# Splitting the first token load by halves of the heads, and the front of an attention and two-MoE kernel

## The reference, cut to what matters

```
scores = scale * x @ state.T            # (8, 8, 512, 32)
a  = softmax over states;  xread = a @ state
a2 = softmax over tokens of scores.T;  sread = a2 @ x
x  = concat(xread, sread)               # 4608 rows of 512
g  = h * clip(h + 3, 0, 6) / 6,  h = x @ w_in;   y = g @ w_out
out = per row: gate * eom * (relu(y @ w1[e]) @ w2[e]),  e = argmax of y @ w_gate
```

## Time and profile before

| | |
|---|---|
| median of 3 runs | 1136.63 us (1136.08 to 1137.5) |
| the profiled execution, its own time | 1139.21 us |
| its span, first to last instruction | 1137.5 us |
| PE busy | 1108.3 us, 97% |
| DVE, ACT, POOL busy | 58%, 42%, 7% |
| mean granted TensorE clock | 0.991 |

### The profile page before, as it was taken

The page is one execution under the profiler, slowest core; times in us unless marked ns, Lnnn a source line. Parts: engine busy times, 40 slices in busy tenths (PEclk is TensorE's granted clock), DMA queues, the critical chain, the costliest instruction groups (busy, mean ns, idle before and its releaser), DMA issues.

```text
span 1137.5 us, 20219 instructions
## 1 busy us (share of the span) xinstructions
PE 1108.3 (97%) x6199; PEld 875.9 (77%) x6200; DVE 659.0 (58%) x1269; ACT 477.0 (42%) x789; POOL 74.7 (7%) x95
## 2 busy tenths in 40 slices
PE   9999999999999999999999997889999999999996
PEld 7777777777777777777777986777888888878885
DVE  6574655565645646546565454775566645657642
ACT  4454434444443444444444444334344423435420
POOL 0000100100001001001000010100111101010011
PEclk9999999999999999999999998999999999999998
DMA  9210211111102101111004088649977754785641
GB/s 366 100 38 1 75 38 37 38 38 54 59 1 75 38 3 73 38 38 38 1 10 121 2 289 261 202 130 279 277 232 228 223 171 140 224 273 175 177 146 60
DMA packets 129794, 135.59 MB, mean 119 GB/s; under 512 B 13999, under 2 KB 107823, under 8 KB 127152
## 3 DMA queue, kind: packets, MB, share of 16 engines
q1 hardware_dynamic: 95056, 87.26, 24.8%
q10 hardware_dynamic: 28896, 29.36, 8.4%
q0 software_dynamic: 5760, 17.90, 4.2%
HBM read 90.06 MB, written 45.47 MB: 119 GB/s over the span
## 4 chain that ended last, share of the span: by engine, by line
PE 86%; DVE 4%; DMA 3%; issue 2%; ACT 2%; SPq 1%; ACTq 1%; DVEq 0%; POOL 0%; POOLq 0%
PE y_ps L962 32%; PE h_ps L944 16%; PE y_ps L1036 15%; PE h_ps L1012 8%; PE y_ps L1012 7%; PE a_ps L919 3%; PE h_ps L934 2%; DMA raw_first<-in_w 2%; ACT we L1209 1%; DMA xg<-buckets 1%; PE a_ps L817 1%; PE a_ps L903 1%; PE a_ps L883 1%; DMA out<-yo,out_row 1%; PE b_ps L825 1%
## 5 line engine op out<-in xcount | busy, mean ns | idle before, releaser
L962 PE MATMUL y_ps<-w_out_hi,hid_hi 128*128 128x512 f32 x512 | 204.7, 400 | 0.0
L962 PE MATMUL y_ps<-w_out_hi,hid_lo 128*128 128x512 f32 x512 | 199.7, 390 | 0.0
L962 PE MATMUL y_ps<-w_out_lo,hid_hi 128*128 128x512 f32 x512 | 199.4, 389 | 0.0
L1036 PE MATMUL y_ps<-we,act_t_hi 128*128 (+1 forms) x608 | 188.6, 392 | 5.1 <-DVE act_t_lo L1632 2.9
L944 PE MATMUL h_ps<-att_hi,mix 128*128 128x512 f32 x512 | 184.1, 403 | 0.1
L1547 DVE SCALAR_TENSOR_TENSOR hid<-hid,h_ps 128x512 f32<-128x512 f32 x128 | 87.7, 685 | 144.8 <-ACT hid L1157 144.8
L1157 ACT ACTIVATE hid<-h_ps,three 128x512 f32<-128x512 f32 x128 | 87.9, 687 | 150.4 <-PE h_ps L944 150.3
L1036 PEld LDWEIGHTS y_ps<-we,act_t_hi 128*128 128x128 f32 x608 | 114.8, 189 | 29.8 <-issue 5.9
L962 PEld LDWEIGHTS y_ps<-w_out_hi,hid_hi 128*128 128x128 f32 x512 | 96.1, 188 | 49.2 <-issue 30.4
L1555 DVE TENSOR_TENSOR hid_lo<-hid,hid_hi 128x512 fp32r<-128x512 f32 x128 | 88.1, 688 | 62.8 <-ACT hid_hi L1164 62.3
L1036 PE MATMUL y_ps<-we,act_t_lo 128*128 (+1 forms) x304 | 119.0, 392 | 0.0
(11 more groups left out here) (249 smaller groups left out, 1517.8 us busy)
## 6 DMA issues: line engine op xcount, KB each, us to landing
raw<-in_w ACTq DMA_DIRECT2D x12, 2048.0 KB, 10.4
hid_mv<-hidden SPq DMA_DIRECT2D x148, 128.0 KB
hidden<-expert_hid SPq DMA_DIRECT2D x70, 256.0 KB
xg<-buckets SPq DMA_DIRECT2D x156, 64.0 KB
xb<-in_x_rows SPq DMA_DIRECT2D x8, 1024.0 KB, 5.0
x_t<-in_x_t SPq DMA_DIRECT2D x7, 1024.0 KB, 4.9
buckets<-pad_row SPq DMA_DIRECT2D x8, 774.0 KB
w_in_raw<-in_w_in SPq DMA_DIRECT2D x4, 1024.0 KB, 13.3
```

The costliest lines, as they stand in the source:

```text
L962: i = pe.matmul(y_ps[:, t, :], hid_of(b, j)[1 + hp][:, t * P:(t + 1) * P], w_out_s[wp][:, j, :], start=(j == 0 and m == 0), stop=(j == KF ...
L1036: i = pe.matmul(y2_ps[:, slot % 2, :], act_t[hp][:, slot % 2, f, :], we[:, bass.ds(w_at + (wp * WPART + KD * F + f * DM), DM)], start=(f = ...
```

## The change

The 1 MB load of the first batch's tokens becomes two loads of 512 KB, one for partitions 0 to 63 (heads 0 to 3) and one for partitions 64 to 127 (heads 4 to 7), with the load of the states between them. The first batch's scores are issued group by group: the four matmuls of group 0 after the first half's load, raising a new semaphore `s1_first`, then the four of group 1 after the second half's load, raising `s1_ps`. TURN 0 of the first batch waits for `s1_first` in place of `s1_ps`. WARM_START goes from 60 to 44 matmuls. Other batches' scores keep their order.

```diff
-    WARM_START, WARM = 60, {0: 75, 3: 55, 8: 30}
+    WARM_START, WARM = 44, {0: 75, 3: 55, 8: 30}
...
-        load_x_t(0)
+        sp.dma_start(x_t[0:D], x_t_dram[0, 0:D]).then_inc(sem("x_t_first"), 16)
         sp.dma_start(keys_of(0), keys[0]).then_inc(sem("first_keys_loaded"), 16)
+        sp.dma_start(x_t[D:2 * D], x_t_dram[0, D:2 * D]).then_inc(sem("x_t_loaded0"), 16)
         load_in(0)
...
+                    x_of = keys_t(a)
+                    if a == 0:
+                        pe.wait_ge(sem("first_keys_loaded"), 16)
+                        for g in range(GROUPS):
+                            pe.wait_ge(sem(("x_t_first", "x_t_loaded0")[g]), 16)
+                            for q in range(H // GROUPS):
+                                i = pe.matmul(bank_ap(g)[NS * q:NS * q + NS, :], keys_of(a)[D * g:D * g + D, q, :],
+                                              x_of[D * g:D * g + D, q, :], start=True, stop=True)
+                            i.then_inc(sem(("s1_first", "s1_ps")[g]), 1)
+                        continue
                     wait(pe, f"x_t_loaded{a % 2}", 16 * (a // 2 + 1))
-                    if a == 0:
-                        pe.wait_ge(sem("first_keys_loaded"), 16)
-                    else:
-                        pe.wait_ge(sem(f"keys_loaded{a // half_b}"), 16)
-                    x_of = keys_t(a)
+                    pe.wait_ge(sem(f"keys_loaded{a // half_b}"), 16)
...
                 elif name == "TURN":
-                    wait(dve, "s1_ps", a + 1)
+                    if a == 0 and n == 0:
+                        dve.wait_ge(sem("s1_first"), 1)
+                    else:
+                        wait(dve, "s1_ps", a + 1)
```

More of the change, by code:

```diff
@@ L873, in side @@
                             wait(pe, *free)
-                    wait(pe, f"x_t_loaded{a % 2}", 16 * (a // 2 + 1))
+                    x_of = keys_t(a)
                     if a == 0:
                         pe.wait_ge(sem("first_keys_loaded"), 16)
-                    else:
-                        pe.wait_ge(sem(f"keys_loaded{a // half_b}"), 16)
-                    x_of = keys_t(a)
+                        for g in range(GROUPS):
[5 more added lines that the diff above has]
+                        continue
+                    wait(pe, f"x_t_loaded{a % 2}", 16 * (a // 2 + 1))
+                    pe.wait_ge(sem(f"keys_loaded{a // half_b}"), 16)
                     for q in range(H // GROUPS):
```

## The result

Six runs of the changed kernel have a median of 1142.13 us (1139.76 to 1145.29), six of the kernel before 1136.58 (1136.08 to 1137.7). The ratio is 1.0047, 95% interval 1.0035 to 1.0060: 0.47% slower, which is 5.3 us of 1136.58; the two medians are 5.55 apart. The forecast was 1137.9 with a range up to 1139.5, so the result is slower than the range allows.

The account below looks back on a forecast made before the run. PE, busy for 97% of the span, was taken to bound the kernel; group 1's scores 1.44 later less 0.16 of slack gave +1.28 on the median 1136.63, so 1137.9 us, whole range 1135.6 to 1139.5.

Parts of the forecast that it names:

- The stretch that matters: The first 24 us of the chain that ended last, claimed to be the only stretch the change touches.
- a front shift is carried to the end: PE has no idle time from 25 to 640 us, so a shift of its start there is carried on whole.
- a load to half the partitions moves about 220 GB/s: First token halves, 64 partitions each: 524 kB take 2.38 us at 220 GB/s, against 1.36 at the full 385.
- PE's path: Front of PE's program: group 1 and the warm-ups queued behind it start 1.44 later, first layer at 20.04 instead of 18.60.
- the landing of the first half: First token load at the front: first half and states land at 5.37, which is 4.60 plus 0.77 for the slower rate.
- the sum: Whole kernel: 1.28 us later at L1157 and to the end, put on the median 1136.63, gives 1137.9.
- 0.16 of slack: PE's spare time at the first-layer matmuls near 19.84 to 20.00, taken off its 1.44 delay to leave 1.28.
- rival 2: The clock falls back in PE's new gap at the front; 3.4 us at 1.2 GHz cost 1.6 more: 1139.5, chance 0.14.
- the new gap of 1.27: PE idle between the two score groups, from 6.58 to 7.85, while waiting for the second half of the tokens.

Follow-up runs that it names:

- halves by pairs: Changed kernel with the first tokens halved by pairs of heads, each load to all 128 partitions, both groups waiting for both: 1143.08 us, ratio 1.0034 to the kernel before.
- the third profile: The changed kernel profiled again with nothing edited, the first of three later single executions: 1144.46 us.
- no gap at all: Changed kernel with 62 warm-ups at the front instead of 44 and 22 more between the score groups: median 1143.66 us, ratio 1.0042 to the kernel before.

## Why the prediction was wrong

**What held.** The stretch that matters, and that a front shift is carried to the end, held: each late front stands unchanged at 657 us. That a load to half the partitions moves about 220 GB/s held: 226 and 220 against the 220 of the earlier trace rows and the 385 of the earlier trace rows (222 to 242 and 191 to 212 in the same windows of the other four profiles). These agree with the Trainium skill's rule (SBUF — State Buffer, "Door 1: The DMA port swizzle") that partitions 0 to 63 reach only 8 of the 16 ports, and the 319 of the halves by pairs, which reach all partitions, agrees too. Group 0's four matmuls took 1.06 against the 1.07 assumed, and the second half took 2.36 after the states (8.63 - 6.27) against 2.38. That PE's path, with 160 warm-ups queued behind group 1's wait, would bind, held too.

**The first term that failed is the landing of the first half.** "The first half and the states land at 5.37" should have been 6.25. The opening was as I assumed, and so was the rate behind it: the first line of each kernel below has the same 48 GB/s, 132 kB by 2.75, although the three issues took 0.60, 0.57 and 0.50 us where the old two took 0.41 and 0.42. The second line reaches to the landing of the states, in the kernel before and in the changed one:

```profile
0.00:2.75 2.75, 1.70 (x17) 1.72 (x19) 0.02 (x1) 1.50 (x3) 1.66 (x15) 1.00 0.36 48
2.75:5.97 3.22, 3.22 (x40) 3.22 (x39) 0.06 (x1) 0.00 (x0) 0.25 (x2) 1.00 0.95 357
...
0.00:2.75 2.75, 1.70 (x17) 1.71 (x19) 0.02 (x1) 1.50 (x3) 1.66 (x15) 1.00 0.27 48
2.75:6.27 3.52, 3.05 (x30) 2.88 (x28) 0.06 (x1) 0.00 (x0) 0.25 (x2) 1.00 1.01 230
```

Before, 132 + 3.22 x 357 = 1282 kB had moved when the states landed, 168 more than the tokens and the states. In the changed kernel it was 132 + 3.52 x 230 = 942 kB, 352 more than the first half and the states (1 MB is 1049 kB, the half 524, the states 66). So the loads behind share the path well before the ones ahead have landed. At 230 GB/s the 352 kB are 1.5 us, where the 168 before were 0.5 at 357; the sum had no term for this. Why it is twice as much with the split is not shown. So group 0 started at 6.32 in the first profile, 0.09 earlier than before and not 0.90 (6.29 to 6.84 in the five), and group 1 at 8.62 to 9.31, 2.2 to 2.9 later and not 1.44. Less 0.16 of slack this is 2.1 to 2.7, 2.5 for the middle one of the five (9.10); the profiles with no gap and no clock loss show 2.8.

**The step that failed most is the one that left the clock out of the sum.** The forecast has no term for it, and rival 2 had a chance of 0.14. The clock fell in five profiles of five. I compared the new gap of 1.27 with a gap of 1.7 that had kept the clock and a 3.4 us stretch with 1.32 us of work that had lost it. But there are two gaps here, 0.51 and 1.30 in the first profile and up to 1.43 and 1.53 in another, close together: the stretch ahead of the fall in the third profile has 1.89 us of work in 3.41. A single gap between fully busy stretches was the wrong neighbour. Where the second gap was filled, or both, the clock did not fall after its rise in any of four profiles; that shows that the fall needs the second gap. It is not the length of one gap: a single one of 1.75 and 1.77 us with 30 warm-ups kept the clock twice. (The gap of 1.56 with the halves by pairs is no such case: the rise came at 6.66, inside it.) Nor is it PE's busy time alone. In the 3.41 us behind the rise PE was busy for 1.67 and 1.69 us in the two executions with 30 warm-ups, which kept the clock, and for 1.30 to 1.89 in the five that lost it. What also differs is the work: in the five, it is in part a group of four score matmuls by itself, which uses 64 of the 128 rows, with a gap on either side. Whether it is the two gaps or this work between them that counts was not tested.

**Its price was right for one stretch and too small for two.** Rival 2's 1.6 us for one slow stretch is what the first two profiles show (group 1 in 1.71 instead of 1.06, the 75 warm-ups in 5.32 instead of 4.36: 0.65 + 0.96). Three of five had two stretches: group 1 takes 1.93 in each and the 75 warm-ups 6.02, 6.52 and 6.40, together 2.5, 3.0 and 2.9 too much. With the late half of each profile added (group 1's start less 6.41 less 0.16), the sums are 3.7, 4.2, 5.3, 5.1 and 5.5. The markers, in the same order, are 3.7, 4.1, 5.2, 5.0 and 5.5 later than before. So these two terms account for the front of every profile, against 5.3 to 5.55 measured in the median.

**The profile of before hid a term.** The clock's rise is not at a fixed time: 4.4 to 6.7 us in the profiles, and 17.0 in one. The prediction removed 16 warm-ups as if the rise stood at 5.1. In two of the profiles it came after the 44 warm-ups had ended (6.66 and 17.0). With the whole load this costs nothing that could be told (1.0006 and 1.0009), so it is not the main cause.

**What stays open.** Behind the marker the time differs by up to 4.0 us between executions of the same kernel, and some variants lie higher than their markers: no gap at all 1.4 us, halves by pairs 2.5 us (3.6 in the median, 1.1 by the marker). Over all 18 profiles it goes with the clock of the expert stage. Between 690 and 810 us the granted clock is 0.50 for two to five stretches of 3.41 us. The five profiles with five such stretches take 480.3 to 483.5 us from the marker to the end, the five with four 479.7 to 480.6, and the eight with two or three 477.1 to 480.4. No run was made to change that clock alone, so it is a correlation, and why one execution has five and another two is not known. Nor was it settled why the second of two 512 KB loads lands late when both reach all partitions, or what the slower executions with 30 warm-ups do.

## What to carry to other kernels

Splitting a load in order to start on a part of it pays only if the part loads at the full rate: halves along the partitions take nearly as long each as the whole did, and delay everything behind them. Count what the loads behind move meanwhile, too. Where an engine's program is in order and padded with work that keeps its clock up, a late wait moves the padding too; and the idle time that it opens can cost about its own length again in clock. So look at all gaps near each other and at the work between them, and not at the longest alone. Where one profile is all there is, ask which of its times would differ in another execution before you trim something to fit it.

## What the runs showed of the hardware

- With two loads of 512 KB to 64 partitions each, 222 to 242 GB/s moved from 3.0 to 5.5 us in the five profiles of the changed kernel (DMA busy share 1.01 to 1.14); with loads to all 128 partitions it was 369 in the same window before, and 387 to 422 later.
- When the states landed, the loads behind them had already moved 168 kB in the first profile of before and 352 kB in the first of the changed kernel.
- The rise of the clock came at 4.35 to 6.66 us in all profiles but one, in which it came at 17.0, though the warm-ups always start at 1.05.
- In all five profiles of the changed kernel the clock fell again: PE had been idle for 0.5 to 1.4 us and then, behind 1.06 us of score matmuls, for 1.3 to 1.5. It stayed down for 3.41 us with PE busy throughout in two, and for 6.83 us with PE fully busy in the latter half in three.
- The granted-clock column reads 1.00 ahead of the first rise; only the spacing of equal matmuls (0.107 or 0.056 us) shows the level there.
